# A linear-attention block with two MLPs: the diagonal term as one factor per token and head, and outputs first in the first five rounds

## The chip, the cores and the metric

The kernel runs on one core of a Trainium2 chip. The metric is the time of one execution in device microseconds. It computes everything in float32 or in float32 split into a high and a low part.

## The reference

For each batch b (2), head h (8) and time step t (768) a state of 48x48 decays and is added to; then two MLP blocks follow. Cut to what matters:

```python
for t in range(S):
    cur = einsum('bhd,bhe->bhde', u * kt, vt)
    y[:, :, t] = einsum('bhd,bhde->bhe', rt, state + cur)
    state = wt[..., None] * state + einsum('bhd,bhe->bhde', kt, vt)
h = gelu(x @ w_in); u, v = h[..., :512], h[..., 512:]
v_s = einsum('ts,bsd->btd', w_sg, layernorm(v) * g_ln) + b_sg[None, :, None]
x = x + (u * v_s) @ w_out
u = x + (relu(x.T @ w_tok1) @ w_tok2).T      # per batch
out = u + relu(u @ w_ch1) @ w_ch2
```

The term with `cur` is the diagonal: at step t it adds `sum_d(r*u*k)` of this token and head, one number, times the 48 values of v.

## The kernel before

The sequence is cut into 12 chunks of 128 tokens (NCH), six per batch (NC). In each chunk the recurrence becomes matmuls: suffix products of w scale k (`kp`, by `backward` and `scale_k`), prefix products scale r (`rp`, by `forward` and `scale_r`). TensorE then computes the scores of a chunk (`scores`), turns kp into rows (`turn_kp`), computes what the chunk adds to the state (`state_products`) and the outputs (`outputs`), which are masked scores times v plus, for all but a batch's first chunk, the old state (`sbd`) times rp. The diagonal goes by TensorE too: `diagonal(n)` there multiplies `rk` = r*k by a block matrix `ubd` of u, 12 matmuls of 32 columns each, so that each head's number stands in all of its 48 rows; VectorE multiplies this by a turned copy of v into `t1`, and its `y_tile` adds `t1` to the outputs.

The program is written out by hand, one row of instructions per engine, with semaphores between. One round is one chunk. In rounds 0 to 4 (below YR = 5) nothing of the MLPs runs: ten range checks of w (`check_range`, on ScalarE) must first be counted (`sum_range` on TensorE, `count_range` on VectorE), upon which GpSimd branches and sets `flag`. From round 5 on, products of the first MLP stand between the chunk's matmuls (table SLOT; `u`, `v` and `sg` are its products with w_in and w_sg), and TAIL has all others. ScalarE evacuates v and u with gelu and makes the high halves of split operands (`xt_high`, `split_high`), GpSimd the low ones (`xt_low`, `split_low`), in the order of their rows in the program. In rounds 0 to 4 ScalarE's iteration n is `take_k(n)` (copies the turned kp into `kn`), `take_state(n-1)` (two copies of the state into `sbd`), the checks of `checks[n]`, `xt_high(n-2)`. `keep_busy` runs matmuls of no use while the first loads are under way.

An engine's instruction waits for its semaphores and holds up everything behind it on that engine:

```python
checks = {0: (2,), 1: (3, 4), 2: (5, 6), 3: (7, 8), 4: (9,)}
def take_k(n):
    act.wait_ge(kn_turned, states(n))
    if n:
        act.wait_ge(ds_done, states(n - 1))
```

## Time and profile before

| | us |
|---|---|
| median of 3 runs (384.88 to 390.32) | 386.17 |
| profiled execution | 387.06 |
| its span, first to last instruction | 385.6 |
| busy: TensorE, GpSimd, VectorE, ScalarE | 364.2, 176.3, 163.2, 105.9 |
| mean granted clock of TensorE | 0.987 of 2.4 GHz |

The profile is of one execution. The busy time is a mean over stages with different limits: in the first 42 us VectorE is nearly always busy, from about 49 us on TensorE is. A timeline row gives an instruction or a run of like ones with its start, its length and, in brackets, the idle time ahead of it on this engine with what ended it. A matmul in float32 leaves two records, a transpose one; their ends are modelled, so the pace is read from start to start. The clock is granted at one of two levels, 2.4 or 1.2 GHz, shown as 1.0 and 0.5.

### The profile page before, as it was taken

What the parts mean: (1) busy time and instruction counts of PE and PEld (TensorE: products, weight loads), DVE (VectorE), ACT (ScalarE), POOL (GpSimd) and SP (SyncE); (2) the same over time, 40 slices, a digit from 0 to 9 for tenths busy, and PEclk for the clock granted to TensorE, in tenths of its full rate; (3) what the DMA queues carried; (4) which work ended last, traced back from release to release, by engine and by line L of the source; (5) the groups of instructions that cost most, each with busy time, mean ns of one, the idle gap of its engine ahead of it and who ended that gap; (6) DMA issues with size and microseconds to landing.
All of it is one profiled execution on the core that took longest, in us unless ns stands there. A gap on an engine that the chain in (4) does not pass through costs nothing.

```text
span 385.6 us, 7208 instructions
## 1 busy us (share of the span) xinstructions
PE 364.2 (94%) x2926; PEld 323.6 (84%) x2926; DVE 163.2 (42%) x293; ACT 105.9 (27%) x197; POOL 176.3 (46%) x181
## 2 busy tenths in 40 slices
PE   6875889999599999999999999999999999999996
PEld 5754778899599989999999999888888888888885
DVE  7997469885044414123432677331013310133110
ACT  4566425565140018340000334320012300033000
POOL 6776499999539998635999930000000000000000
PEclk9999899999799999999999999999999999999999
DMA  8999639821202020030214300000100001000001
GB/s 226 288 310 276 194 111 243 242 92 43 83 2 82 2 81 2 3 82 2 82 43 125 122 2 2 0 0 3 53 27 2 0 0 56 27 0 2 0 30 53
DMA packets 13954, 28.82 MB, mean 75 GB/s; under 512 B 1888, under 2 KB 6496, under 8 KB 13920
## 3 DMA queue, kind: packets, MB, share of 16 engines
q1 hardware_dynamic: 13920, 28.34, 25.3%
q8 instruction: 24, 0.39, 0.4%
q14 instruction: 10, 0.08, 0.1%
HBM read 25.98 MB, written 2.36 MB: 73 GB/s over the span
## 4 chain that ended last, share of the span: by engine, by line
PE 84%; issue 1%; ACT 1%; DVE 1%; DVEq 0%; ACTq 0%
PE bank L1109 77%; PE bank L1188 3%; PE bank L1205 1%; PE bank L1129 1%; PE bank L1239 1%; PE bank L1139 1%; PE bank L1151 1%; ACT uT L779 0%; ACT sg_hi L835 0%; ACT win_hi L835 0%; DVE bank L962 0%; ACT xT_hi L816 0%; DVE xr L962 0%; DVE xr L1043 0%; DVE st L954 0%
## 5 line engine op out<-in xcount | busy, mean ns | idle before, releaser
L790 ACT ACTIVATE ha_hi<-bank 128x512 fp32r<-128x512 f32 x36 | 21.5, 598 | 100.5 <-PE bank L1109 100.5
L1035 DVE SCALAR_TENSOR_TENSOR ha_lo<-bank,ha_hi 128x512 fp32r<-128x512 f32 x36 | 24.9, 692 | 49.7 <-ACT ha_hi L790 49.7
L1109 PE MATMUL bank<-u2T_hi,c_hi 128*128 128x512 f32 x108 | 42.1, 389 | 0.0
L1109 PE MATMUL bank<-u2T_lo,c_hi 128*128 128x512 f32 x108 | 42.0, 389 | 0.0
L1109 PE MATMUL bank<-ha_hi,c_lo 128*128 128x512 f32 x108 | 42.0, 389 | 0.0
L1109 PE MATMUL bank<-ha_lo,c_hi 128*128 128x512 f32 x108 | 42.0, 389 | 0.0
L1109 PE MATMUL bank<-ha_hi,c_hi 128*128 128x512 f32 x108 | 42.0, 389 | 0.0
L1109 PE MATMUL bank<-u2T_hi,c_lo 128*128 128x512 f32 x108 | 42.0, 389 | 0.0
L1109 PE MATMUL bank<-sg_hi,z_lo 128*128 128x384 f32 x96 | 33.5, 349 | 4.1 <-issue 4.1
L1109 PE MATMUL bank<-sg_hi,z_hi 128*128 128x384 f32 x96 | 33.2, 346 | 0.0
L1109 PE MATMUL bank<-sg_lo,z_hi 128*128 128x384 f32 x96 | 33.2, 346 | 0.0
L1044 DVE TENSOR_TENSOR xr<-bank,xr 128x512 f32<-128x512 f32 (+1 forms) x9 | 5.9, 661 | 57.9 <-PE bank L1109 57.9
L1109 PEld LDWEIGHTS bank<-ha_hi,c_lo 128*128 128x128 f32 x108 | 20.3, 188 | 4.2
L1109 PEld LDWEIGHTS bank<-ha_lo,c_hi 128*128 128x128 f32 x108 | 20.3, 188 | 4.2
L1109 PEld LDWEIGHTS bank<-u2T_lo,c_hi 128*128 128x128 f32 x108 | 20.3, 188 | 4.2
L1109 PEld LDWEIGHTS bank<-u2T_hi,c_lo 128*128 128x128 f32 x108 | 20.3, 188 | 4.2
L1109 PEld LDWEIGHTS bank<-u2T_hi,c_hi 128*128 128x128 f32 x108 | 20.3, 188 | 4.2
L1109 PEld LDWEIGHTS bank<-ha_hi,c_hi 128*128 128x128 f32 x108 | 20.3, 188 | 4.1
L574 POOL TENSOR_TENSOR c_lo<-raw,c_hi 128x768 fp32r<-128x768 f32 x12 | 23.1, 1928 | 1.0
L1109 PEld LDWEIGHTS bank<-sg_hi,z_lo 128*128 128x128 f32 x96 | 18.8, 196 | 4.6 <-issue 4.6
L1020 DVE SCALAR_TENSOR_TENSOR tmp<-bank,gln,bsg 128x384 f32<-128x384 f32 x16 | 9.9, 617 | 24.5 <-PE bank L1109 21.5
L538 POOL TENSOR_SCALAR gt_hi<-tmp 128x384 fp32r<-128x384 f32 x16 | 9.5, 592 | 21.7 <-DVE tmp L1024 21.7
(136 smaller groups left out, 838.0 us busy)
## 6 DMA issues: line engine op xcount, KB each, us to landing
krT<-in_kr_turned SPq DMA_DIRECT2D x12, 448.0 KB, 8.7
vn<-in_v_both SPq DMA_DIRECT2D x12, 416.0 KB, 9.6
raw<-in_moe_w_ch SPq DMA_DIRECT2D x12, 384.0 KB, 3.1
raw<-in_moe_w_sg SPq DMA_DIRECT2D x6, 384.0 KB, 4.6
out<-xr SPq DMA_DIRECT2D x8, 256.0 KB, 2.0
raw<-in_moe_w_in SPq DMA_DIRECT2D x4, 384.0 KB, 12.4
raw<-in_moe_w_tok SPq DMA_DIRECT2D x4, 384.0 KB, 3.5
wz<-in_w_turned SPq DMA_DIRECT2D x6, 225.8 KB, 7.9
```

Source lines behind the costliest of these rows:

```text
L538: return nc.gpsimd.tensor_scalar(dst, src, 1.0, 1.0, ALU.mult, ALU.mult)
L574: gp.tensor_tensor(lo, raw_view(piece, hi), hi.bitcast(F32), ALU.subtract).then_inc(w_split, 1)
L790: sc.activation(ha[0][:, i, :], bank[:, :], ACT.Relu).then_inc(act_out, 1)
L1020: ve.scalar_tensor_tensor(tmp[:, i % 2, :], bank[:, 0:HALF], gln[:, dt:dt + 1], bsg[:, at_], ALU.mult, ALU.add).then_inc(dve_out, 1)
L1035: ve.scalar_tensor_tensor(ha[1][:, i, :], bank[:, :], 0.0, ha[0][:, i, :].bitcast(F32), ALU.max, ALU.subtract).then_inc(dve_out, 1)
L1044: ve.tensor_tensor(dst[:, done:WIDE], bank[:, done:WIDE], dst[:, done:WIDE], ALU.add).then_inc(dve_out, 1)
L1109: ins = te.matmul(dst, left[l], right[r], start=first and l == 1, stop=last and (l, r) == (0, 0))
L1129: ins = te.matmul(bs[i][:, tile(p)], kp[q, n % 2, p, :], rp[q, n % RR, p, :], start=True, stop=True)
L1139: ins = te.transpose(b2[:, QP * p:QP * p + QP], kp[0:QP, n % 2, p, :], ident[0:QP, 0:QP])
L1151: ins = te.matmul(b1[q, D * p:D * p + D], kn[:, p, q], vn[:, n % VR, QP * p + HP * i:QP * p + HP * i + D], start=True, stop=True)
L1188: ins = te.matmul(yb[32 * g:32 * g + 32, tile(a)], left, right, start=first, stop=last)
L1205: ins = te.matmul(dg_bank(n)[32 * g:32 * g + 32, tile(a)], ubd[0:QP, p, 32 * j:32 * j + 32], rk[0:QP, n % 2, p, :], start=True, stop=True)
```

## The change

- The diagonal. TensorE's `diagonal(n)` is now 4 matmuls with `rk` as the stationary side and 2 columns of `ubd` as the moving one. They give one number per token and head (8 columns, `dg_cols`). VectorE multiplies v by it, spread over 48 columns each, into `vd`. TensorE adds `vd` to the outputs by three full 128x128 matmuls against the identity, at the head of `outputs(n)`, into the same accumulation. `y_tile` and `t1` are gone; in rounds 0 to 4 ScalarE's new `take_y` copies the outputs to `xr`, later `x_tile` reads the bank itself. The second, turned copy of v is no longer loaded: a transfer of v has 256 KB instead of 416 KB.
- Scores and masked scores have two buffers each in these rounds, so `mask(n)` waits for the outputs of n-2.
- The order in rounds 0 to 4. On TensorE: outputs(n), state_products(n), diagonal(n+1), scores(n+1), turn_kp(n+1); before: scores(n), turn_kp(n), diagonal(n), state_products(n), outputs(n). On ScalarE: take_y(n-1), take_state(n-1), take_k(n+1), checks[n].
- The tables. v(0,0) moves from round 5 to 6 and every later job of SLOT by one place; sg(0,0) moves to the head of TAIL. GpSimd makes kp and rp of chunk 6 right after `flag`, ahead of the low halves of w_in pieces 2 and 3, and rp of chunk 0 comes from GpSimd instead of VectorE. The warm-up is 14 narrow and 22 full matmuls instead of 54 narrow ones.

```diff
@@ -39,13 +39,15 @@
...
-DUMMIES = 54
+NARROW, FULL = 14, 22
...
-VW = NP * QP
+VP = 2 * HP
+VW = NP * VP
...
+DCOL = NP * D
...
@@ -66,15 +68,15 @@
...
 SLOT = {
-    5: [("u", 0, 0), ("u", 0, 2), ("v", 0, 0)],
-    6: [("v", 0, 1), ("v", 0, 2)],
-    7: [("v", 0, 3), ("v", 0, 4)],
-    8: [("v", 0, 5), ("u", 0, 4)],
-    9: [("u", 0, 6), ("u", 0, 1)],
-    10: [("u", 0, 3), ("u", 0, 5)],
-    11: [("u", 0, 7), ("sg", 0, 0)],
+    5: [("u", 0, 0), ("u", 0, 2)],
+    6: [("v", 0, 0), ("v", 0, 1)],
+    7: [("v", 0, 2), ("v", 0, 3)],
+    8: [("v", 0, 4), ("v", 0, 5)],
+    9: [("u", 0, 4), ("u", 0, 6)],
+    10: [("u", 0, 1), ("u", 0, 3)],
+    11: [("u", 0, 5), ("u", 0, 7)],
 }
-TAIL = ([("sg", 0, i) for i in range(1, 8)] + [("v", 1, i) for i in range(6)] + [("out", 0, i) for i in range(6)]
+TAIL = ([("sg", 0, i) for i in range(8)] + [("v", 1, i) for i in range(6)] + [("out", 0, i) for i in range(6)]
...
@@ -338,20 +340,20 @@
...
-        heads, b1, b2, bs, by = ps[0][0:QP, 0:RUN // 2], ps[1], ps[2], ps[3:5], ps[5]
-        bc = b2[:, 0:CHECKS]
-
-        def y_bank(n):
-            return ps[6] if n < YR and n % 2 else by
+        heads, b1, b2, by = ps[0][0:QP, 0:RUN // 2], ps[1], ps[2], ps[5]
+        bc = ps[7][:, 0:CHECKS]
+
+        def dg_cols(n):
+            return b1[:, DCOL:DCOL + H] if n else ps[3][:, 0:H]
+
+        def score_banks(n):
+            return ps[6:8] if n < YR and n % 2 == 0 else ps[3:5]
...
@@ -668,9 +670,8 @@
...
                 gp.tensor_copy(flag[:, :], nhalf[:, :]).then_inc(flagged, 1)
+                scale(YR + 1)
                 split_low("w_in", 2)
-                split_low("w_in", 3)
-                scale(YR + 1)
                 for n in range(YR, NCH):
                     chunk(n)
...
@@ -698,7 +699,7 @@
...
-            scale_k(0)
+            scale(0)
...
@@ -802,6 +803,11 @@
...
+            def take_y(n):
+
+                act.wait_ge(av_done, n + 1)
+                sc.copy(x_cols(n), tiles(by)).then_inc(y_done, 1)
...
@@ -834,31 +840,34 @@
...
-            high = {4: [("w_in", 0), ("w_in", 2)], 5: [("w_in", 3)], 6: [("w_in", 1)], 7: [("w_sg", 0), ("w_sg", 1)],
-                    8: [("w_sg", 2)], 9: [("w_sg", 3)], 10: [("w_sg", 4)], 11: [("w_sg", 5)]}
+            high = {4: [("w_in", 0), ("w_in", 2)], 5: [("w_in", 3)], 6: [("w_in", 1)], 7: [("w_sg", 0)], 8: [("w_sg", 1)],
+                    9: [("w_sg", 2)], 10: [("w_sg", 3), ("w_sg", 4)], 11: [("w_sg", 5)]}
...
-            for q, e in ((slice(0, D), slice(0, D)), (slice(HP, QP), slice(D, 2 * D))):
-                sc.copy(ubd[q, :, e], ucol[q, :].rearrange("q (p a) -> q p a", a=1).to_broadcast([D, NP, D])
-                        ).then_inc(u_made, 1)
+            for q, e in ((slice(0, D), 0), (slice(HP, QP), 1)):
+                sc.copy(ubd[q, :, e:e + 1], ucol[q, :].rearrange("q (p a) -> q p a", a=1)).then_inc(u_made, 1)
...
             checks = {0: (2,), 1: (3, 4), 2: (5, 6), 3: (7, 8), 4: (9,)}
+            take_k(0)
             for n in range(YR):
-                take_k(n)
                 if n:
+                    take_y(n - 1)
                     take_state(n - 1)
+                if (n + 1) % NC < NC - 1:
+                    take_k(n + 1)
                 for i in checks[n]:
                     check_range(i)
                 if n > 1:
                     xt_high(n - 2)
                 for piece in high.get(n, ()):
                     split_high(*piece)
+            take_y(YR - 1)
             take_state(YR - 1)
             for n in range(YR, NCH):
-                if n % NC < NC - 1:
+                if n > YR and n % NC < NC - 1:
                     take_k(n)
...
@@ -919,26 +928,22 @@
...
-            def scale_first_r():
-
-                wait_ring(dve, krT_in, 0)
-                dve.wait_ge(pre_done, 1)
-                ve.tensor_tensor(rp[0:QP, 0], krT[0][0:QP, 1], runs(pre, 0), ALU.mult).then_inc(rp_done, 1)
...
             def diagonal(n):
 
                 wait_ring(dve, v_in, n)
                 dve.wait_ge(dg_done, n + 1)
-                if n:
-                    dve.wait_ge(y_done, n)
-                ve.tensor_tensor(t1[:, :], dg_bank(n)[:, 0:C], vn[:, n % VR, VW:VW + C], ALU.mult).then_inc(t1_done, 1)
+                if n > 1:
+                    dve.wait_ge(av_done, n - 1)
+                ve.tensor_tensor(vd[:, n % 2, :].rearrange("s (p i d) -> s p i d", p=NP, i=2),
+                                 dg_cols(n).rearrange("s (p i a) -> s p i a", p=NP, a=1).to_broadcast([PART, NP, 2, D]),
+                                 vn[:, n % VR, :].rearrange("s (p i x) -> s p i x", p=NP, i=2)[:, :, :, 0:D], ALU.mult).then_inc(vd_done, 1)
...
             def mask(n, i):
 
                 dve.wait_ge(qk_done, n + 1)
-                if n:
-                    dve.wait_ge(av_done, n)
-                ve.tensor_tensor(am[:, :, :].rearrange("s (p i) t -> s i p t", i=2)[:, i, :, :], pairs(bs[i]),
+                if n > 1:
+                    dve.wait_ge(av_done, n - 1)
+                ve.tensor_tensor(am[:, n % 2].rearrange("s (p i) t -> s i p t", i=2)[:, i, :, :], pairs(score_banks(n)[i]),
...
@@ -954,18 +959,11 @@
...
-            def y_tile(n):
-
-                dve.wait_ge(av_done, n + 1)
-                dve.wait_ge(t1_done, n + 1)
-                src = tiles(y_bank(n))
-                ve.tensor_tensor(x_cols(n) if n < YR else src, src, tiles(t1), ALU.add).then_inc(y_done, 1)
...
             def x_tile(n):
 
                 if n == YR:
                     dve.wait_ge(flagged, 1)
-                dve.wait_ge(y_done, n + 1)
+                dve.wait_ge(av_done, n + 1)
...
@@ -1057,17 +1055,16 @@
...
             backward(0)
             forward(0)
-            scale_first_r()
             backward(1)
             forward(1)
             for n in range(YR):
                 mask(n, 0)
                 mask(n, 1)
+                if n == 0:
+                    diagonal(0)
                 backward(n + 2)
                 forward(n + 2)
-                if n:
-                    y_tile(n - 1)
-                diagonal(n)
+                diagonal(n + 1)
                 if n == YR - 1:
                     count_range()
                 state(n)
@@ -1075,19 +1072,16 @@
...
                 for b, i in v_jobs(n):
                     stats(b, i)
-                diagonal(n)
-                y_tile(n)
                 x_tile(n)
+                if n + 1 < NCH:
+                    diagonal(n + 1)
                 if n % NC < NC - 1:
                     state(n)
-            take_job("sg", 0, 0)
...
@@ -1121,8 +1115,11 @@
...
-                if n:
-                    pe.wait_ge(masked, 2 * n)
+                if n > 1:
+                    pe.wait_ge(masked, 2 * (n - 1) if n <= YR else 2 * n)
+                if n == 1:
+                    pe.wait_ge(vd_done, 1)
+                bs = score_banks(n)
...
@@ -1145,10 +1140,11 @@
...
                 if n:
                     pe.wait_ge(st_done, states(n - 1))
+                    pe.wait_ge(vd_done, n + 1)
...
@@ -1158,11 +1154,12 @@
...
                 if n > YR:
                     pe.wait_ge(x_out, n - YR)
-                elif n == YR:
+                elif n:
                     pe.wait_ge(y_done, n)
-                elif n >= 2:
-                    pe.wait_ge(y_done, n - 1)
-                inner, yb = n % NC > 0, y_bank(n)
+                inner = n % NC > 0
+                pe.wait_ge(vd_done, n + 1)
+                for a in range(KC):
+                    te.matmul(by[:, tile(a)], vd[:, n % 2, tile(a)], ident[:, :], start=a == 0, stop=False)
                 if inner:
                     pe.wait_ge(sbd_done, 2 * states(n - 1))
                 pe.wait_ge(masked, 2 * (n + 1))
@@ -1172,20 +1169,20 @@
...
-                        here = old + [(vn[:, n % VR, c:c + 32], am[:, h, :]) for c, h in new]
-                        todo += [(a, left, right, e == 0, e == len(here) - 1) for e, (left, right) in enumerate(here)]
+                        here = old + [(vn[:, n % VR, c:c + 32], am[:, n % 2, h, :]) for c, h in new]
+                        todo += [(a, left, right, a == KC - 1 and e == len(here) - 1) for e, (left, right) in enumerate(here)]
...
-                            a, left, right, first, last = part
-                            ins = te.matmul(yb[32 * g:32 * g + 32, tile(a)], left, right, start=first, stop=last)
+                            a, left, right, last = part
+                            ins = te.matmul(by[32 * g:32 * g + 32, tile(a)], left, right, start=False, stop=last)
...
@@ -1195,22 +1192,17 @@
...
-                    pe.wait_ge(t1_done, n)
-                if n >= YR:
-                    pe.wait_ge(kn_copied, states(n))
-                    pe.wait_ge(ok_counted, 1)
-                for a in range(KC):
-                    for g in range(4):
-                        p, j = divmod(4 * a + g, 3)
-                        ins = te.matmul(dg_bank(n)[32 * g:32 * g + 32, tile(a)], ubd[0:QP, p, 32 * j:32 * j + 32],
-                                        rk[0:QP, n % 2, p, :], start=True, stop=True)
-                        yield
+                    pe.wait_ge(vd_done, n)
+                    if n > 1:
+                        pe.wait_ge(st_done, states(n - 2))
+                for p in range(NP):
+                    ins = te.matmul(dg_cols(n)[:, 2 * p:2 * p + 2], rk[0:QP, n % 2, p, :], ubd[0:QP, p, :], start=True, stop=True)
                 ins.then_inc(dg_done, 1)
...
             def sum_range():
 
                 pe.wait_ge(checked, CHECKS)
-                pe.wait_ge(kn_copied, states(YR - 1))
+                pe.wait_ge(masked, 2 * YR)
                 te.matmul(bc, ones[:, :], acc[:, :], start=True, stop=True).then_inc(ok_summed, 1)
...
@@ -1291,10 +1281,12 @@
...
-            def keep_busy(m):
-
-                for i in range(m):
+            def keep_busy(narrow, full):
+
+                for i in range(narrow):
                     te.matmul(ps[6][32 * (i % 4):32 * (i % 4) + 32, 0:PART], ident[:, 0:32], ident[:, :], start=True, stop=True)
+                for i in range(full):
+                    te.matmul(ps[6][:, 0:PART], ident[:, :], ident[:, :], start=True, stop=True)
...
@@ -1302,25 +1294,31 @@
...
-            keep_busy(DUMMIES)
+            keep_busy(NARROW, FULL)
+            scores(0)
+            turn_kp(0)
+            diagonal(0)
             for n in range(YR):
-                scores(n)
-                turn_kp(n)
-                rest_of(diagonal(n))
-                rest_of(state_products(n))
                 if n == YR - 1:
                     sum_range()
                 rest_of(outputs(n))
+                rest_of(state_products(n))
+                diagonal(n + 1)
+                scores(n + 1)
+                if (n + 1) % NC < NC - 1:
+                    turn_kp(n + 1)
             for n in range(YR, NCH):
-                scores(n)
-                if n % NC < NC - 1:
-                    turn_kp(n)
+                if n > YR:
+                    scores(n)
+                    if n % NC < NC - 1:
+                        turn_kp(n)
                 for job in round_jobs(n):
                     product(*job)
-                rest_of(diagonal(n))
                 rest_of(outputs(n))
                 if n % NC < NC - 1:
                     rest_of(state_products(n))
+                if n + 1 < NCH:
+                    diagonal(n + 1)
             for job in TAIL:
...
@@ -1354,10 +1352,9 @@
...
-        t = a.reshape(B, NP, 2, NC, PART, D).transpose(0, 3, 4, 1, 2, 5).reshape(NCH, PART, NP, 2, D)
-        t = _np.concatenate([t[..., 0, :], _np.zeros_like(t[..., 0, :HP - D]), t[..., 1, :]], axis=3)
-        c = a.reshape(B, H, NC, PART, D).transpose(0, 2, 1, 4, 3).reshape(NCH, KC, PART, PART).transpose(0, 2, 1, 3)
-        return _np.concatenate([t.reshape(NCH, PART, VW), c.reshape(NCH, PART, C)], axis=2)
+        t = a.reshape(B, H, NC, PART, D).transpose(0, 2, 3, 1, 4).reshape(NCH, PART, H, D)
+        t = _np.concatenate([t, _np.zeros_like(t[..., :HP - D])], axis=3)
+        return _np.ascontiguousarray(t.reshape(NCH, PART, VW))
...
```

TensorE's row in the program from the last of outputs(1) to the first of outputs(2), before (L1188 is outputs, L1129 scores, L1139 turn_kp, L1205 the old diagonal, L1151 state products):

```order
L1188 MATMUL bank<-rp,sbd 32x128
L1188 MATMUL bank<-am,vn 32x128 x4
L1129 MATMUL bank<-rp,kp 128x128 x8
L1139 MATMUL bank<-ident,kp 128x112 x4
L1205 MATMUL bank<-rk,ubd 32x128 x12
L1151 MATMUL bank<-vn,kn 64x48
```

And of the change, from the last state products of chunk 1 on (L1147 is state products, L1199 the new diagonal, L1126 scores, L1134 turn_kp, L1162 the injects of vd, L1185 outputs):

```order
L1147 MATMUL bank<-vn,kn 64x48
L1147 MATMUL bank<-vn,kn 48x48
L1199 MATMUL bank<-ubd,rk 128x2 x4
L1126 MATMUL bank<-rp,kp 128x128 x8
L1134 MATMUL bank<-ident,kp 128x112 x4
L1162 MATMUL bank<-ident,vd 128x128 x3
L1185 MATMUL bank<-rp,sbd 32x128 x4
L1185 MATMUL bank<-am,vn 32x128 x4
```

Scores and turn_kp of chunk 2 now stand behind outputs and state products of chunk 1, and the injects of chunk 2 stand behind turn_kp(2).

ScalarE's row before, from take_k(1) on (L732 is take_k, L740 and L741 take_state, L758 and L760 checks, L816 xt_high):

```order
L732 COPY kn<-bank 128x448
L740 COPY sbd<-st 48x4x48
L741 COPY sbd<-st 48x4x48
L758 ACTIVATE junk,ok<-wz,ok 112x1024
L760 ACTIVATE junk,ok<-wz,ok 112x1024
L732 COPY kn<-bank 128x448
L740 COPY sbd<-st 48x4x48
L741 COPY sbd<-st 48x4x48
L758 ACTIVATE junk,ok<-wz,ok 112x1024
L760 ACTIVATE junk,ok<-check_w,ok 128x1152
L816 CAST xT_hi<-xr 128x3x128
```

And of the change, from take_k(0) and take_k(1) on (L733 is take_k, L809 take_y, L741 and L742 take_state, L759 and L761 checks):

```order
L733 COPY kn<-bank 128x448 x2
L761 ACTIVATE junk,ok<-wz,ok 112x1024
L809 COPY xr<-bank 128x3x128
L741 COPY sbd<-st 48x4x48
L742 COPY sbd<-st 48x4x48
L733 COPY kn<-bank 128x448
L759 ACTIVATE junk,ok<-wz,ok 112x1024
L761 ACTIVATE junk,ok<-wz,ok 112x1024
L809 COPY xr<-bank 128x3x128
L741 COPY sbd<-st 48x4x48
L742 COPY sbd<-st 48x4x48
L733 COPY kn<-bank 128x448
```

The first two `kn` copies are take_k(0) and take_k(1); take_y(0) and take_state(0) now stand behind take_k(1) and a check, where take_state(0) stood behind take_k(1) alone; from take_y(1) on there is a pair of checks in between.

## Rows read from the trace of the kernel before

**Rows 1.** The page: TensorE's busy time, share of the span, instructions.
```profile
PE 364.2 (94%) x2926; PEld 323.6 (84%) x2926; DVE 163.2 (42%) x293; ACT 105.9 (27%) x197; POOL 176.3 (46%) x181
```

**Rows 2.** Timeline of VectorE: start us, length us, engine, line, operation, tiles, shapes.
```profile
21.23 1.28 DVE L941 TENSOR_TENSOR am<-bank,cmask 128x512 f32<-128x512 f32 x2
...
25.08 0.53 DVE L962 TENSOR_TENSOR xr<-bank,t 128x384 f32<-128x384 f32 x1
...
26.88 1.28 DVE L941 TENSOR_TENSOR am<-bank,cmask 128x512 f32<-128x512 f32 x2
```

**Rows 3.** Timeline of TensorE; in brackets the idle time before, and its releaser.
```profile
8.59 1.16 PE L1129 MATMUL bank<-rp,kp 48*128 48x128 f32 x16 [2.02 <-DVE rp L926]
...
30.48 0.41 PE L1205 MATMUL bank<-rk,ubd 112*32 112x128 f32 x4 [2.47 <-issue]
...
39.05 0.77 PE L1151 MATMUL bank<-vn,kn 128*64 128x48 f32 x11 [3.17 <-issue]
...
49.34 0.47 PE L1109 MATMUL bank<-win_hi,xT_lo 128*128 128x512 f32 x1 [1.85 <-issue]
```

**Rows 4.** The chain of waits in order of time: start us, us, what.
```profile
61.42 0.59 PE bank L1151 x14
62.01 1.09 PE bank L1129 x16
63.11 0.53 PE bank L1139 x4
63.64 4.14 PE bank L1109 x18
67.78 0.79 PE bank L1205 x24
68.57 1.54 PE bank L1188 x56
...
80.56 3.17 PE bank L1109 x18
...
97.76 3.58 issue
101.34 6.10 PE bank L1109 x18
```

**Rows 5.** Timeline of ScalarE in round 3.
```profile
27.27 0.53 ACT L732 COPY kn<-bank 128x448 f32<-128x448 f32 x1 [2.15 <-PE bank L1139]
27.70 0.35 ACT L740 COPY sbd<-st 48x192 f32<-48x192 f32 x1
...
28.45 1.26 ACT L758 ACTIVATE junk<-check_w,ok 128x1152 bf16<-128x1152 f32 x1
...
31.08 0.50 ACT L816 CAST xT_hi<-xr 128x384 fp32r<-128x384 f32 x1
```

**Rows 6.** Timeline of GpSimd.
```profile
25.20 1.00 POOL L611 TENSOR_TENSOR xT_lo<-xr,xT_hi 128x384 fp32r<-128x384 f32 x1 [2.47 <-ACT xT_hi L816]
...
28.43 1.28 POOL L585 TENSOR_TENSOR rk<-krT 112x512 f32<-112x512 f32 x1
...
41.63 0.18 POOL L670 COPY flag<-nhalf 128x1 f32<-128x1 f32 x1 [1.04 <-DVE oki L979]
...
47.44 1.80 POOL L574 TENSOR_TENSOR win_lo<-raw,win_hi 128x768 fp32r<-128x768 f32 x1 [3.85 <-ACT win_hi L835]
...
99.44 1.81 POOL L574 TENSOR_TENSOR sg_lo<-raw,sg_hi 128x768 fp32r<-128x768 f32 x1
```

**Rows 7.** Weight loads by form up to 110 us: count, busy us, mean ns.
```profile
L1129 PEld LDWEIGHTS bank<-rp,kp 48*128 48x128 f32 x192 | 11.7, 187 | 3.7 <-issue 3.5
...
L1205 PEld LDWEIGHTS bank<-rk,ubd 112*32 112x32 f32 x288 | 7.4, 109 | 8.2 <-issue 7.4 <-POOL rk L585 0.4
```

**Rows 8.** Timeline of TensorE at the first transposes of x1t.
```profile
168.92 2.13 PE L1239 MATMUL bank<-ident,xr 128*128 128x128 f32 x18
```

**Rows 9.** A stretch: us, busy PE, PEld, DVE, ACT, POOL, granted clock, DMA.
```profile
39.60:43.03 3.43, 3.43 (x66) 2.90 (x61) 1.17 (x6) 1.21 (x3) 2.39 (x3) 0.58 0.69 210
```

More of the change, by code:

```diff
@@ L182, in build @@
     suf = put("suf", [PART, 2, RUN + 4])
-    vn = put("vn", [PART, VR, VW + C])
+    vn = put("vn", [PART, VR, VW])
     pre = put("pre", [PART, RUN + 4])
@@ L187, in build @@
     kn = put("kn", [PART, NP, QP])
-    am = put("am", [PART, H, PART])
+    am = put("am", [PART, 2, H, PART])
     sbd = put("sbd", [PART, 2, NP, 2 * D])
     st = put("st", [PART, NP, D])
-    t1 = put("t1", [PART, C])
+    vd = put("vd", [PART, 2, C])
     ucol = put("ucol", [PART, NP])
-    ubd = put("ubd", [PART, NP, 2 * D])
+    ubd = put("ubd", [PART, NP, 2])
     cmask = put("cmask", [PART, PART])
@@ L252, in build @@
         table_in = sem("table_in")
[L253 removed]
+        rp_done, rk_done, vd_done, flagged = sem("rp_done"), sem("rk_done"), sem("vd_done"), sem("flagged")
         xt_hi, xt_split, u2_hi, u2_split = sem("xt_hi"), sem("xt_split"), sem("u2_hi"), sem("u2_split")
@@ L391, in load_v @@
                     sp.wait_ge(ds_done, states(n - VR))
-                    sp.wait_ge(t1_done, n - VR + 1)
+                    sp.wait_ge(vd_done, n - VR + 1)
                 sp.dma_start(vn[:, n % VR, :], v_both[n]).then_inc(v_in[n % VR], 16)
@@ L435, in _ @@
             load_raw(2)
-            later = {5: [3], 6: [4, 5], 7: [6], 8: [7], 9: [8], 10: [9, 10], 11: [11, 12, 13, 14]}
+            later = {5: [3], 6: [4, 5], 7: [6], 8: [7], 9: [8], 10: [9], 11: [10, 11, 12, 13, 14]}
             for n in range(4, NCH):
@@ L641, in split_gated @@
                                  ).then_inc(g_split, 1)
-            low = {6: [("w_in", 1)], 7: [("w_sg", 0), ("w_sg", 1)], 8: [("w_sg", 2)], 9: [("w_sg", 3)],
-                   10: [("w_sg", 4)], 11: [("w_sg", 5)]}
+            low = {5: [("w_in", 3)], 6: [("w_in", 1)], 7: [("w_sg", 0)], 8: [("w_sg", 1)], 9: [("w_sg", 2)],
+                   10: [("w_sg", 3), ("w_sg", 4)], 11: [("w_sg", 5)]}
             def scale(n):
@@ L1077, in _ @@
                 mask(n, 1)
-                if n == YR:
-                    y_tile(n - 1)
                 if n + 2 < NCH:
@@ L1174, in parts @@
                         p, j = divmod(4 * a + g, 3)
-                        v0 = QP * p + 32 * j
+                        v0 = VP * p + 32 * j
                         old = [(sbd[0:QP, n % 2, p, 32 * j:32 * j + 32], rp[0:QP, n % RR, p, :])] if inner else []
@@ L1224, in free_bank @@
                 elif JOB[job][0] < EARLY:
-                    pe.wait_ge(ok_counted, 1)
-                    pe.wait_ge(y_done, YR - 1)
-                    pe.wait_ge(t1_done, YR)
+                    pe.wait_ge(masked, 2 * YR)
                 else:
```

7 lines of the change are left out of this document (1 added, 6 removed).

## The prediction

> **What bounds the kernel now.** I read the page first: TensorE (PE) is busy 94% of a span of 385.6 us, so what is left to move is what keeps PE waiting or makes it slow [rows 1]. The profiled execution took 387.06 us, 1.5 more than its span; the median of the runs is 386.17.
>
> The first 42 us are not PE's. VectorE (DVE) runs without a hole from mask(2) at 21.23 to mask(3) at 26.88, 5.65 us a round; y_tile at 25.08 is 0.53 of it [rows 2]. PE waits inside its rounds: 2.47 us before 30.48 and 3.17 us before 39.05, both put down to issue [rows 3]. After the second wait the clock was granted at 0.58 between 39.60 and 43.03, that is, mostly at 1.2 GHz instead of 2.4 [rows 9]. The fifth round ends with GpSimd (POOL) setting `flag` at 41.63, behind DVE's count of the range [rows 6]. Call this moment F: before it no product of the MLP may start.
>
> From F on the chain of waits is nearly all PE, and one round reads: state products 0.59, scores 1.09, turning 0.53, two v products 4.14, the old diagonal 0.79, outputs 1.54; two u products are 3.17 [rows 4]. There is one hole, 3.58 us at 97.76, while POOL ends the splits of `w_sg`, and behind it sg(0,0) takes 6.10 us for 18 matmuls of the shape that the u products do in 3.17: the clock is at its low level again [rows 4]. sg(0,1) starts at 101.34 + 6.10 + 0.79 + 1.54 = 109.77, 68.1 us after F. From there PE has no hole worth naming, and the change leaves that part alone.
>
> So the time after is 387.06 plus the shift of F, plus the change of the 68.1 us.
>
> **The change part by part.** *Round 0 to 4, the new order.* The order of ScalarE (ACT) is what matters most. Outputs(n) now wait for take_y(n-1) and take_state(n-1) on ACT. These stand behind take_k(n) and the range checks of iteration n-1. Take_k(n) waits for turn_kp(n), which stands in PE's row behind scores(n), diagonal(n), state_products(n-1) and outputs(n-1). This closes a loop through both engines with nothing running in parallel: turn_kp(n), take_k(n), checks, take_y, take_state, outputs(n), state products(n), diagonal(n+1), scores(n+1), turn_kp(n+1). Before, the checks stood behind take_state and hence behind what outputs waited for, in the shadow of DVE's 5.65 us.
>
> Prices of ACT's half: take_k to the next copy 0.43 (27.27 to 27.70), the two copies of take_state 0.75, a pair of checks 2.63 (28.45 to 31.08), so 1.3 for one, and xt_high 0.5 [rows 5]. Take_y is new there, a copy of 128x384 like xt_high; of each 0.45 counts, up to the next start. With 0.1 for the hand-over to PE, round 1 (one check) is 0.43+1.3+0.45+0.85 = 3.0 us, round 2 (two checks) 4.3, round 3 (and xt_high) 4.8.
>
> Prices of PE's half: outputs 1.54, state products 0.59, scores 1.09, turning with the hand-over 0.64 [rows 4], and the new diagonal. This is 4 matmuls (8 records) whose moving side is 2 columns and whose stationary side is 128, so the weight loads set it. No row shows this alone. Below: the state products' 16 records in 0.59 us, 37 ns each with 48 to 64 columns to load [rows 4], 0.3 us. Above: 8 loads of 187 ns one behind the other, 1.5 us. Loads of 32 and of 128 columns last 109 and 187 ns [rows 7], 0.8 ns for each further column, so 128 columns cost 0.10 us and with a little overhead 0.11: 0.9 us, which I take. PE's half is then 1.54+0.59+0.9+1.09+0.64 = 4.76.
>
> Start: scale_r(0) goes to POOL behind scale_k(0), and the warm-up is 14 narrow and 22 full matmuls instead of 54 narrow. Scores(0) began at 8.59 [rows 3]; kp(0) and rp(0) are now ready at about 8.2, the wider warm-up may hold PE until 10.7 if the clock is low for most of it, and I take 9.2. From there scores 1.09, turning 0.53, diagonal 0.9, VectorE's vd 0.9 with both hand-overs, inject 0.75, outputs(0) 0.88, state products 0.59, diagonal 0.9, scores 1.09, turning 0.64: T1 = 17.5, where Tn is the end of turn_kp(n).
>
> T2 = 17.5+3.0+4.8 = 25.3. T3 = 25.3+4.3+4.8 = 34.4. In round 3 POOL comes in: rk(4) stands behind xt_low(0) and scale(4). Before, from the xT_lo row at 25.20 to the start of rk at 28.43 are 3.2 us, and rk itself is 1.28 [rows 6]; xt_high(0) starts at T3+3.05 and takes 0.55, so rk(4) ends (0.55+0.1+3.2+1.28) at T3+8.15, and diagonal(4) starts there instead of at T3+6.9. T4 = 34.4+8.2+0.9+1.09+0.64 = 45.2. Round 4: PE's sum_range stands ahead of outputs(4) and waits for check 9, which is behind a pair of checks, xt_high(1), take_y and take_state: 45.2+0.43+2.6+0.45+0.45+0.75+1.4 = 51.3. Then sum 0.5, inject 0.75, outputs 1.54, state products 0.59, diagonal 0.9: 55.6; VectorE's vd 0.65 and count 0.6; POOL 0.7 later: F = 57.5. It was 41.63: **+15.9 us**. A round of 8 to 11 us stands where 5.65 stood, although DVE is rid of y_tile's 0.53 and PE's issue waits (2.47, 3.17) have room to vanish in it. What hid the checks was DVE's 5.65; that cover is gone.
>
> *The clock.* PE now idles some 3.5 us in round 2, 4 in round 3 and 6 in round 4. The wait of 3.17 us brought the low level in the trace, that of 2.47 did not. A stretch of 3.4 us at 1.2 GHz costs 1.7 us of PE's work; in round 3 it mostly hides behind POOL. I add **+3.4** for rounds 2 and 4; the bounds are 0 and 7, the latter if the low level lasts as it did at sg(0,0), 2.9 us lost each time.
>
> *After F.* PE per round: the old diagonal goes (-0.79), the new one comes (+0.9), and three full 128x128 matmuls against the identity in fp32 (6 records). The x1t transposes are full 128x128 too: 18 in 2.13 us, of which 0.27 is the last one's own length, so 0.109 us from one to the next [rows 8]; 6 of these are 0.65, with a change of the array's shape 0.75. So +0.86 in each round. Here the notes speak against the change: the Trainium skill, TensorEngine Tiling (Array Packing), Key Properties, says that changing the tiling mode drains the engine, and the injects add one change per round. The rows show no idle time at such changes, only scores' 1.09 where 8 steps of 0.11 would be 0.9; by the rule each round would pay up to 0.2 more than my 0.1, another 1 us in all.
>
> Counting from F with POOL's new order (scale(6) 2.3, low(w_in,2) 1.8, rk 1.25, two xt_low 1.9, low(w_in,3) 1.8): v(0,0) starts at F+9.4, against 7.7 before, at 49.34 [rows 3]. Rounds 6 to 11 on PE: 4.14+0.75+0.88+0.59+0.9+1.09+0.53 = 8.9 for round 6; 9.5 for 7 and for 8; 8.6 for 9; 8.0 for 10; 3.17+0.75+1.54 = 5.5 for 11. sg(0,0) may start at F+59.4. POOL ended its last `w_sg` split at 101.25, 59.6 us after F, and 3.85 of these it waited for ACT, ahead of 47.44 [rows 6]. In its new order scale(6) fills that wait, so about 56 are left. It is done 3 us before PE asks, the hole of 3.58 us closes, PE stays at the high level and sg(0,0) takes 3.17. sg(0,1) starts at F+62.6 instead of F+68.1: **-5.5 us**.
>
> The v transfers shrink from 416 KB to 256 KB; they only were late where DVE and PE ran at the old pace, so I give nothing for it. Sum: 387.06+15.9+3.4-5.5 = 400.9, and by the median 400.
>
> **The rivals.** (1) The loop through ACT binds and the clock falls: 400. (2) It binds, the clock stays high in these rounds: 396.6. For it speaks that 2.47 us of idling did nothing; against it that 3.17 us did. (3) It binds, but small prices are too high: a diagonal at 0.55 instead of 0.9 takes 0.35 off ten times on the path, and with the high clock 393 comes out, about the edge of 2%. (4) Faster: the checks do not delay outputs, since ACT would reach take_y and take_state before PE has ended scores(n). Then VectorE sets the rounds at 5.1 us, F comes 2.7 earlier for five rounds and some 2 more for the issue waits, and with -5.5 the time is 377. It decides if ACT's half is under about 1 us; the rows make it 3 to 4.8, in program order, so I give it little. (5) The two sides cancel, within 2% in all: F would have to shift by no more than 13, which needs each round shorter than my sum by 1 us.
>
> **How the numbers follow.** (1) 0.57, (2) 0.18, (3) and (5) together 0.20, of which 0.03 lies just outside 2%, (4) 0.05. About 2% is what a measurement of this kernel can tell. Slower by over 2% means above 393.9: 0.78; within: 0.17; faster: 0.05. Range: low, 400.9 with no cost of the clock (-3.4), the diagonal cheap (-3.5) and a start 1 us sooner is 393, and two more for round errors 391; high, the clock at 7 and a diagonal at 1.2 is 407.
>
> **What would show it.** ACT's row in rounds 1 to 4 should read kn, checks, (xT_hi), xr, sbd, sbd with no gap but one ahead of kn of some 4 us; PE should wait for ACT's sbd or xr ahead of outputs; `flag` should come at 55 to 62 us instead of 41.63. After F: v(0,0) 9.4 later, no hole ahead of sg(0,0), sg(0,1) some 62.6 after F, the new diagonal at 0.9 and the injects at 0.75. The prediction is wrong if F stands under 50, or if PE's rounds after F are as short as before.

## The result and the profile after

The changed kernel takes 409.25 us (median of 4 runs, 408.65 to 412.32); the kernel before took 387.03 beside it. The ratio is 1.060, its 95% interval 1.056 to 1.065 (it is taken from fast runs alone and so is a little above the quotient of the two medians): slower, as forecast, but above the 400.0 and above the end of the range, 407. The profiled execution is 408.65 us with a span of 407.1.

The page of the changed kernel, TensorE (PE) and its clock in 40 slices of 10.2 us:

```profile
PE   8787638999999999999999999999999999999996
...
PEclk9967667999999999999999999999999999999999
```

Slices 3 to 7, from 20 to 71 us, hold the loss: the clock's digits are 6 and 7 there, and PE's busy share falls to 6 and 3 tenths in slices 5 and 6. (The digits are tenths, of full speed or of the slice.) What follows is as full as before. `flag` on GpSimd (POOL), which answers to 41.63 in [rows 6], and what it waited for:

```profile
67.22 0.18 POOL L672 COPY flag<-nhalf 128x1 f32<-128x1 f32 x1 [3.64 <-DVE oki L977]
```

F, the moment of `flag`, moved by 25.6 us and lies outside the 55 to 62 that the prediction named as its sign; from F to the start of sg(0,1), 68.1 us before, it is 64.2 (67.22 to 131.4), and what is behind differs by 0.1. So 25.6 - 3.9 - 0.1 = 21.6 is the difference of the profiled executions, 408.65 - 387.06.

ScalarE (ACT) in round 2, from its timeline, which answers to [rows 5]:

```profile
28.75 0.53 ACT L733 COPY kn<-bank 128x448 f32<-128x448 f32 x1 [7.94 <-PE bank L1134]
29.31 1.15 ACT L759 ACTIVATE junk<-wz,ok 112x1024 bf16<-112x1024 f32 x1
...
31.73 0.46 ACT L809 COPY xr<-bank 128x384 f32<-128x384 f32 x1
32.09 0.35 ACT L741 COPY sbd<-st 48x192 f32<-48x192 f32 x1
32.47 0.35 ACT L742 COPY sbd<-st 48x192 f32<-48x192 f32 x1
```

And the rows of PE's timeline that had an idle time ahead of them, from round 1 to the sum of the range (L1162 is the inject at the head of outputs, L1206 the sum of the range):

```profile
20.30 1.62 PE L1162 MATMUL bank<-ident,vd 128*128 128x128 f32 x6 [2.18 <-issue]
...
32.29 1.62 PE L1162 MATMUL bank<-ident,vd 128*128 128x128 f32 x6 [3.57 <-issue]
...
44.06 1.62 PE L1162 MATMUL bank<-ident,vd 128*128 128x128 f32 x6 [4.09 <-issue]
...
58.69 0.60 PE L1206 MATMUL bank<-ok,ones 128*128 128x10 f32 x2 [6.14 <-ACT junk L759]
```

This is the loop that was forecast: PE stands still while ACT does kn, checks and xr, and ACT's only gap is ahead of kn. That gap is 7.94 us, where some 4 were forecast; in e2 below, at full clock, it is 5.30. The inject at 32.29 starts 0.1 us after xr ends (31.73 + 0.46), so "issue" hides a wait for xr. It does not wait for the two sbd copies, the second of which starts after it. What was not forecast is the 1.62 of the injects: they run at half the clock. Windows of the changed kernel, drawn near the edges of these stretches (columns: busy time of each engine, then the clock, the share of DMA and GB/s):

```profile
19.80:26.60 6.80, 6.30 (x83) 5.44 (x84) 1.71 (x3) 0.99 (x4) 3.59 (x3) 0.54 1.04 294
30.05:36.90 6.85, 4.61 (x69) 4.05 (x71) 2.15 (x4) 2.71 (x7) 0.00 (x0) 0.54 0.48 139
43.70:50.50 6.80, 6.43 (x84) 5.58 (x84) 1.41 (x2) 0.87 (x3) 4.47 (x4) 0.54 0.17 51
53.90:64.20 10.30, 5.51 (x79) 4.79 (x80) 2.13 (x4) 6.81 (x14) 7.24 (x6) 0.53 0.09 23
67.60:71.00 3.40, 3.34 (x12) 3.37 (x13) 2.91 (x6) 2.21 (x5) 3.21 (x3) 0.58 0.25 69
```

Five stretches at 1.2 GHz, 34 us in all, where the kernel before had one of 3.4 us ahead of F [rows 9] and one of 6.8 us behind it, at sg(0,0) (granted 0.54 from 101.06 to 107.90). The chain of waits of the changed kernel for round 3, the end of round 4, and the rounds behind F:

```profile
44.06 1.62 PE bank L1162 x6
45.68 3.15 PE bank L1185 x56
48.83 1.02 PE bank L1147 x14
...
67.66 4.69 PE bank L1103 x18
72.35 0.67 PE bank L1162 x6
73.02 1.68 PE bank L1185 x56
74.69 0.98 PE bank L1199 x8
...
128.24 6.79 PE bank L1103 x38
```

Inject 1.62 instead of 0.67, outputs 3.15 instead of 1.68, state products 1.02 instead of 0.59: 2.85 us lost in round 3 on the path. At 128.24 sg(0,0) follows without a hole, where [rows 4] had 3.58 us of waiting and a slow product; its row in the chain holds sg(0,0) and what follows it.

### The profile page after: what moved, and what is told of

Read it like the earlier page. It is cut to its first block, busy times and chain, and to the rows that moved or that the text cites. A ratio compares the mean times of both kernels' runs of the same rounds, so it can differ in the third digit from the quotient of the medians.

```text
span 407.1 us, 6871 instructions
## 1 busy us (share of the span) xinstructions
PE 384.3 (94%) x2770; PEld 345.0 (85%) x2770; DVE 157.2 (39%) x280; ACT 107.7 (26%) x202; POOL 177.5 (44%) x182
## 4 chain that ended last, share of the span: by engine, by line
PE 94%; issue 3%; ACT 1%; DVE 0%; POOL 0%; POOLq 0%; DVEq 0%; ACTq 0%
PE bank L1103 73%; PE bank L1185 6%; PE bank L1126 3%; PE bank L1162 3%; PE bank L1199 3%; PE bank L1147 2%; PE bank L1289 1%; PE bank L1134 1%; PE bank L1229 1%; ACT junk L759 1%; PE bank L1287 0%; DVE vd L937 0%; PE bank L1206 0%; POOLq L716 0%; DVE xr L1041 0%
## 5 line engine op out<-in xcount | busy, mean ns | idle before, releaser
L1103 PE MATMUL bank<-sg_hi,z_lo 128*128 128x384 f32 x96 | 32.3, 336 | 0.0
L1103 PE MATMUL bank<-sg_hi,z_hi 128*128 128x384 f32 x96 | 32.1, 334 | 0.0
L1103 PE MATMUL bank<-sg_lo,z_hi 128*128 128x384 f32 x96 | 32.1, 334 | 0.0
L613 POOL TENSOR_TENSOR xT_lo<-xr,xT_hi 128x384 fp32r<-128x384 f32 x12 | 13.4, 1117 | 27.7 <-ACT xT_hi L822 27.7
L1162 PE MATMUL bank<-ident,vd 128*128 128x128 f32 x72 | 13.2, 332 | 10.6 <-issue 9.8
L1185 PE MATMUL bank<-am,vn 128*32 128x128 f32 x384 | 22.0, 318 | 0.0
```

Source lines behind the costliest of these rows:

```text
L613: gp.tensor_tensor(lo, x_cols(g), hi.bitcast(F32), ALU.subtract).then_inc(xt_split, 1)
L1103: ins = te.matmul(dst, left[l], right[r], start=first and l == 1, stop=last and (l, r) == (0, 0))
L1162: te.matmul(by[:, tile(a)], vd[:, n % 2, tile(a)], ident[:, :], start=a == 0, stop=False)
L1185: ins = te.matmul(by[32 * g:32 * g + 32, tile(a)], left, right, start=False, stop=last)
```

## Experiments

**Is it the loop through ScalarE?** e1_take_k puts take_k(n) behind take_state(n-1), as the kernel before had it.

```diff
-                if (n + 1) % NC < NC - 1:
-                    take_k(n + 1)
+                if n:
+                    take_k(n)
```

> The changed kernel with one line of ScalarE's order in rounds 0 to 4 altered: behind take_state(n-1) stands take_k(n) instead of take_k(n+1), so the checks no longer stand between a turn_kp and the outputs that follow it. If the loop through ScalarE is what costs (theory): a round is turning, 0.7 for the inject, outputs 1.68, state products 0.6, diagonal 0.98, scores 1.09, turning 0.53, about 5.6 us instead of 10.6 to 12.6, no idle of over 2 us before outputs, the clock stays high until round 4, flag comes at about 45 us instead of 67.2, and the time is about 387. If the outputs-first order of TensorE or the new diagonal's price is what costs (rival): 400 or more.

390.46 us (ratio 1.016, 1.008 to 1.024), `flag` at 48.73 instead of 67.22. VectorE's masks (L946) now come every 5.98 us, in its timeline:

```profile
26.18 1.28 DVE L946 TENSOR_TENSOR am<-bank,cmask 128x512 f32<-128x512 f32 x2
...
31.02 0.56 DVE L937 TENSOR_TENSOR vd<-bank,vn 128x384 f32<-128x384 f32 x1 [0.91 <-PE bank L1199]
...
32.16 1.28 DVE L946 TENSOR_TENSOR am<-bank,cmask 128x512 f32<-128x512 f32 x2
```

One moved line takes off 18.8 of the 22.2 us by the medians, or 4.4 of the 6.0% by the ratios, each to the kernel before that ran beside it. The rest came in above the 387 I expected: vd waits 0.91 us a round for the new diagonal, scores(0) starts at 10.74 behind the wide warm-up, and the sum waits 2.43 us for check 9. The clock is low for short stretches too, granted at 0.51 from 14.60 to 18.00, behind a wait of 0.81 us, and at 0.50 from 42 to 45, behind the wait of the sum.

e3_small_checks shortens the same half of the loop in another way: checks 2 to 9 read 8 columns, so most of the range check is left out.

```diff
+                if i > 1:
+                    src, dst = (src[:, 0:1, 0:8], dst[:, 0:1, 0:8]) if i < NC else (src[:, 0:8], dst[:, 0:8])
```

> The changed kernel with checks 2 to 9 reading 8 columns of w instead of 1024 or 1152; their number, order and semaphores stay. It leaves out most of the range check. A check falls from 1.28 to some 0.45 us. If the checks in the loop are the cover that was lost (theory), the eight of them give back 6.6 us, and more (up to 8) where the idle before outputs gets short enough for the clock to stay high: 394 to 403. If the loop binds by something else on ScalarE or GpSimd (rival): 408 to 410.

400.24 us (1.044, 1.031 to 1.057), `flag` at 57.64, 9.6 us earlier, and the idle times ahead of the injects are 1.33, 1.88 and 2.29. That checks delay outputs is shown. The clock still fell in four of five rounds: behind the wait of 1.33 us it was granted at 0.51 from 19.50 to 22.80.

**Is the rest the clock?** e2_fill puts matmuls of no use where PE waits for ACT, 9, 15, 17 and 26 of them behind turn_kp(1) to turn_kp(4); nothing on ACT's side changes.

```diff
                 if (n + 1) % NC < NC - 1:
                     turn_kp(n + 1)
+                    for _ in range(FILL[n]):
+                        te.matmul(score_banks(n)[0][:, 0:PART], ident[:, :], ident[:, :], start=True, stop=True)
```

> The changed kernel with matmuls of no use (9, 15, 17 and none, full 128x128) behind turn_kp(1) to turn_kp(4), 26 behind the last, in the wait for ScalarE; the order is left alone. If the low clock is what made the rounds longer than their sum at the high clock (theory): the injects take 0.67 instead of 1.6, outputs 1.7 instead of 3.1, the rounds 7.8, 9.1 and 10.8 instead of 10.6, 11.3 and 12.6, and the time is 400 to 402. If ScalarE's half is longer than I priced it and the clock matters little (rival): 408 to 410.

403.58 us (1.050, 1.042 to 1.058); `flag` at 59.51, 7.7 us earlier with more work on PE. The profiled execution, 401.06 us, is 7.6 below that of the changed kernel; the median is above the 400 to 402 that I expected. PE's idle rows in it:

```profile
20.04 0.91 PE L1163 MATMUL bank<-ident,vd 128*128 128x128 f32 x6 [0.15 <-issue]
...
39.28 0.91 PE L1163 MATMUL bank<-ident,vd 128*128 128x128 f32 x6 [0.28 <-issue]
43.44 1.05 PE L1200 MATMUL bank<-ubd,rk 112*128 112x2 f32 x8 [0.99 <-POOL rk L588]
```

The injects are at full speed, and the wait for GpSimd's rk(4), which the prediction had put into round 3, shows once PE is fast.

e8_fill_first fills only the first wait, the one of 2.18 us: FILL is (9, 0, 0, 0).

> The changed kernel with filler matmuls only in round 1 (9 full matmuls behind turn_kp(1)), so that TensorE does not idle the 2.18 us ahead of the injects of outputs(1). Theory (each idle stretch brings its own 6.8 us at 1.2 GHz): the low stretch from 19.8 to 26.6 us goes and the later three stay, flag comes some 2.5 us earlier than 67.2, the time is 405.5 to 407.5. Rival (the low level comes from the whole of rounds 0 to 4 being lightly used, and one filled wait is made up by an earlier or longer low stretch): as many low stretches as before, flag within 1 us of 67.2, 408.5 to 410.

406.93 us (1.055, 1.047 to 1.063), `flag` at 63.35, 3.9 us earlier; 0.3 of these were there already at scores(0) (9.38 instead of 9.69). The first stretch of its windows, and PE's row at the second wait:

```profile
19.80:26.60 6.80, 5.82 (x107) 5.09 (x106) 3.73 (x8) 1.45 (x5) 3.60 (x3) 1.00 1.04 330
```

```profile
29.34 1.62 PE L1163 MATMUL bank<-ident,vd 128*128 128x128 f32 x6 [3.57 <-issue]
```

The first fence is the window, the second PE's row. The clock is 1.00 where it was 0.54; the second wait, untouched, still brings an inject at 1.62, and the third one does too (40.58). So each wait brings its own stretch. Not all of the 3.9 us reached the end, 2.4 of them did in the profiled executions: behind F the low stretch moved from the first u pair (3.38 us instead of 4.69) to the v pair (5.95 instead of 4.13), and ahead of that stands an issue wait of 0.95.

**Would another order of PE close the loop elsewhere?** e4_scores_first puts diagonal(n+1), scores(n+1), turn_kp(n+1) ahead of outputs(n).

```diff
-                rest_of(outputs(n))
-                rest_of(state_products(n))
                 diagonal(n + 1)
                 scores(n + 1)
                 if (n + 1) % NC < NC - 1:
                     turn_kp(n + 1)
+                rest_of(outputs(n))
+                rest_of(state_products(n))
```

> The changed kernel with TensorE's order in rounds 0 to 4 turned back in part: diagonal(n+1), scores(n+1), turn_kp(n+1), then outputs(n), state_products(n), and state products wait for vd(n+1) since they share its bank; ScalarE's order is left as the change has it. Theory: take_k(n+1) then waits for the state products of n, the loop is take_k 0.5, a pair of checks 2.6, xt_high 0.45, take_y and take_state 1.2, outputs 1.7, state products 0.6, some 7.2 us a round instead of 11.3, and the idle before outputs is short enough for the high clock: about 394 to 398. Rival, that TensorE's order is of no account beside ScalarE's: 405 or more.

A miss: 412.35 us (1.071, 1.062 to 1.079), `flag` at 71.12. The rival's number came true, but TensorE's order is of account: it made things worse. PE's timeline in it:

```profile
47.80 1.87 PE L1199 MATMUL bank<-ubd,rk 112*128 112x2 f32 x8 [8.29 <-POOL rk L587]
65.42 1.87 PE L1199 MATMUL bank<-ubd,rk 112*128 112x2 f32 x8 [8.42 <-POOL rk L587]
```

rk stands behind xt_low on GpSimd, xt_low waits for xt_high, which stands behind the checks on ACT, and these behind take_k. The loop closes through three engines; I had followed only two.

**What stands behind F?** e5_old_pool is e1 with GpSimd's order of before behind `flag` (low halves of w_in pieces 2 and 3 ahead of scale(6)).

> The kernel of e1_take_k with GpSimd's order behind flag as it was before the change: the low halves of w_in pieces 2 and 3 first, then kp and rp of chunk 6, and no split in chunk 5. It isolates the new order on GpSimd. Theory of the prediction, that scale(6) ahead of the splits is needed to fill GpSimd's wait: scores(6) and all behind it start later or GpSimd ends its splits later, a hole opens ahead of sg(0,0), 391 to 398. Rival: since the high half of piece 3 is early now, the wait is gone either way, v(0,0) starts some 1.8 us earlier than the 10.1 us after flag, and the time is 388 to 389.

391.62 us (1.013, 1.010 to 1.016), not to be told from e1's. It lies in the range of the theory, but without its hole. The wait behind `flag` that the prediction built on, 3.85 us ahead of a half of w_in [rows 6], does not come back, it is 0.52; a wait of 3.85 stands later, ahead of a half of w_sg, and e1 has one of 3.58 in that place. PE has no hole ahead of sg(0,0): the first fence is GpSimd's timeline, the second the chain.

```profile
52.25 1.83 POOL L576 TENSOR_TENSOR win_lo<-raw,win_hi 128x768 fp32r<-128x768 f32 x1 [0.52 <-ACT win_hi L842]
...
83.84 1.83 POOL L576 TENSOR_TENSOR sg_lo<-raw,sg_hi 128x768 fp32r<-128x768 f32 x1 [3.85 <-ACT sg_hi L842]
...
108.28 1.84 POOL L576 TENSOR_TENSOR sg_lo<-raw,sg_hi 128x768 fp32r<-128x768 f32 x1
```

```profile
109.60 1.68 PE bank L1186 x56
111.28 0.89 PE bank L1104 x4
```

The last split ends 60.4 us after `flag`, in e1 60.0, and sg(0,0) starts 1.2 us behind it. So in this kernel GpSimd's order is not what closes the hole. e7_tables_only takes the kernel before and gives it the change's tables alone (SLOT, TAIL, the orders of the splits and raw loads, and GpSimd's order behind `flag`); diagonal, rounds 0 to 4 and warm-up stay.

```diff
-    5: [("u", 0, 0), ("u", 0, 2), ("v", 0, 0)],
-    6: [("v", 0, 1), ("v", 0, 2)],
+    5: [("u", 0, 0), ("u", 0, 2)],
+    6: [("v", 0, 0), ("v", 0, 1)],
...
-TAIL = ([("sg", 0, i) for i in range(1, 8)]
+TAIL = ([("sg", 0, i) for i in range(8)]
```

> The kernel before with the change's tables alone: SLOT and TAIL (sg(0,0) at the head of TAIL), GpSimd's order behind flag, the tables of high and low halves and of raw loads. The diagonal, the order of rounds 0 to 4 and the warm-up stay as before. Theory: flag stays at about 41.6, the hole of 3.6 us and the low clock at sg(0,0) go, and with the old diagonal (0.79 us a round instead of 0.98+0.67) sg(0,1) starts some 60 us after flag instead of 68: 378 to 382. Rival, that the hole closed only because flag came so late that loads and splits were ready: 385 or more.

382.48 us (0.988, 0.981 to 0.994): the tables are the good part of the change, though `flag`, at 43.55, came 1.9 us later than before. Its chain has, in place of 3.58 us of waiting and 6.10 of a slow sg(0,0):

```profile
98.36 1.54 PE bank L1186 x56
99.90 1.86 issue
101.75 10.32 PE bank L1107 x58
```

PE comes to sg(0,0) 56.4 us after `flag`, about as before (56.1), but with outputs(11) behind it by then, and GpSimd's last split ends 58.1 us after `flag` instead of 59.6. The products behind the wait of 1.86 us ran at full clock.

e6_diag_twice measures the new diagonal alone: it is issued twice for chunks 7 to 11.

```diff
-                for p in range(NP):
+                for p in tuple(range(NP)) * (2 if n > YR + 1 else 1):
```

> The changed kernel with the four matmuls of the new diagonal issued twice for chunks 7 to 11, where TensorE has no hole. If one diagonal is worth the 0.98 us that stands between its start and the next one's in the trace, five more cost 4.9 us: 413.5 to 415. If weight loads of 128 columns hide under other work as the trace of the kernel before would allow (0.3 us), 1.5 us: about 410.8. An inject would cost nothing more in either.

417.14 us (1.080, 1.071 to 1.089), more than either expected. Its chain of waits:

```profile
94.68 1.88 PE bank L1199 x16
...
98.18 5.71 PE bank L1103 x18
...
118.31 1.64 PE bank L1126 x16
```

And two of its windows:

```profile
98.00:100.00 2.00, 2.00 (x7) 1.56 (x6) 2.00 (x4) 1.92 (x4) 0.00 (x0) 0.55 0.00 0
118.60:122.00 3.40, 3.40 (x25) 3.17 (x22) 2.28 (x5) 1.76 (x4) 3.40 (x4) 0.51 0.23 89
```

Two diagonals are 1.88, so a further diagonal costs 0.90 and the first 0.98: five make 4.5 us of the 8.1 by which the span grew. The rest is the clock: behind two of the five double diagonals it fell for 3.4 us with PE busy all the time. The v pair took 5.71 instead of 4.13, and in the other place scores, turning and a u pair 1.6 more. With 0.4 by which `flag` was later that is the 8.1.

**A version that beats both?** b1 is e1 with check 9 in iteration 3, xt_high ahead of the checks, the count ahead of diagonal(5) on VectorE, and 12 full matmuls in the warm-up instead of 22.

```diff
-NARROW, FULL = 14, 22
+NARROW, FULL = 14, 12
...
-            checks = {0: (2,), 1: (3, 4), 2: (5, 6), 3: (7, 8), 4: (9,)}
+            checks = {0: (2,), 1: (3, 4), 2: (5, 6), 3: (7, 8, 9), 4: ()}
...
-                diagonal(n + 1)
                 if n == YR - 1:
                     count_range()
+                diagonal(n + 1)
```

> The kernel of e1_take_k with check 9 in iteration 3, xt_high ahead of the checks, VectorE's count of the range ahead of diagonal(5), and 12 full warm-up matmuls instead of 22. Theory: TensorE's 2.4 us wait ahead of the range sum and the low clock behind it go, flag no longer waits for outputs(4), state products and diagonal(5), and comes at 41 to 44 us instead of 48.7: 384 to 388. Rival: the product cannot start before scores(5) are done anyway, and the time stays within 1.5 us of e1_take_k's.

383.67 us (0.992, 0.988 to 0.996), `flag` at 41.03, as in the kernel before. Four things changed at once, and none of them is priced alone. b2 moves diagonal(n+1) ahead of outputs(n) too, and vd(n+1) behind the masks:

> The kernel of b1 with diagonal(n+1) ahead of outputs(n) on TensorE and vd(n+1) right behind the masks on VectorE, so that VectorE does not wait 0.9 us a round for it. Theory: the rounds fall from 5.98 us to 5.1 to 5.3, some 3 us less than b1: 381 to 385. Rival: rk(n+1) from GpSimd comes too late for the earlier place in rounds 2 to 4, and nothing or less is gained.

A miss again: 388.64 us (1.004, 1.002 to 1.006). In the profiled execution, the slowest of the ten (391.34), PE waits for GpSimd at once:

```profile
12.81 1.05 PE L1199 MATMUL bank<-ubd,rk 112*128 112x2 f32 x8 [2.14 <-POOL rk L587]
```

c1 puts b1's checks, xt_high and count on e7:

> The kernel before with the changed tables (382.5 us when it ran) and three more steps off the path to the flag: check 9 with those of round 3, the high half of x ahead of the checks, the count of the range ahead of the diagonal on VectorE. In that run the count waited 1.37 us for TensorE's sum, which waited for check 9. Theory: flag comes 1.5 to 2.5 us earlier than 43.55 and the time is 380 to 381.5. Rival: a late issue of TensorE or the low clock in rounds 1 to 4 sets the flag, and it stays within 1 us: 382 to 383.5.

381.96 us (0.989, 0.985 to 0.992), not to be told from e7. The theory missed; the rival's time is near, but `flag` came 1.5 us later than in e7 and not within 1. The profiled execution is the slowest of the ten (384.45), and GpSimd's timeline in it shows a third reason:

```profile
42.74 1.82 POOL L574 TENSOR_TENSOR win_lo<-raw,win_hi 128x768 fp32r<-128x768 f32 x1
45.01 0.18 POOL L670 COPY flag<-nhalf 128x1 f32<-128x1 f32 x1 [0.45 <-issue]
```

`flag` no longer waits for the count but stands behind a split on its own engine. Issue waits of 3.74 and 2.31 us on PE in rounds 2 and 3 stand ahead of that; that they made it late is argued, not shown. The fastest kernels here, c1, e7 and b1, are 1.1, 1.2 and 0.8% faster than before. That is less than 2%, though each interval lies below 1, and the runs do not rank the three. The first two keep the old diagonal.

## Why the prediction was wrong in size

**The loop: right.** With the waits filled (e2) the loop can be read without the clock: kn starts at 17.91, 25.86, 35.22 and 46.15, and 17.5, 25.3, 34.4 and 45.2 were forecast for T1 to T4. Two errors in it cancelled, by luck. The inject (0.67) was left out of PE's half of 4.76, where it belongs in every round; and the two state copies (0.75) were charged to ACT's half, though they run under the inject, since only the products behind it read the state: kn at 28.75 to the inject at 32.29 is 3.5 us, not 4.3. Round 4 from kn to the sum, 6.1, came out as forecast (52.59 to 58.69). In e2 the 26 matmuls held the sum up, to 7.25 us; with 6.1 its F would be 58.4, and 57.5 was forecast.

**The clock: the step that failed.** It was priced at +3.4 with a bound of 7, for rounds 2 and 4, because an idle time of 2.47 us in the kernel before had brought nothing and one of 3.17 had. Here 2.18 us in round 1 brought the low level (in e3 even 1.33 us did), and e8 shows that this first wait alone moved F by 3.9 us, or 3.6 without the earlier start. Four waits brought four stretches, of 6.8 us three times and 10.3 once, not 3.4 each. F came at 67.22 instead of 57.5 + 3.4 = 60.9; against 58.4 the clock cost 8.8 us ahead of F, where 3.4 stood (0.25 of the 8.8 is a later start than in e2, 9.69 instead of 9.44). The reading was made from two idle times, and the first wait of the changed kernel contradicts it. The row that should have warned me is sg(0,0) in [rows 4]: 2.9 us lost after one hole. I named it as a bound for two rounds instead of taking it for all four.

That round 3 would hide its part behind GpSimd failed too: in the changed kernel rk(4) ended at 48.17 and the slow outputs at 48.8, so PE itself was late.

**The sum.** The loop gave 0.9 us more than forecast, the clock 5.4 and the part behind F 1.6, less 0.1 behind sg(0,1): together the 7.8 us between 400.9 and the profiled execution's 408.65.

**After F: -3.9 instead of -5.5.** v(0,0) started 10.1 us behind F, not 9.4. In e8, with the first u pair at full clock (3.38 instead of 4.69), it is 9.7, so 0.4 is the slow u pair; the other 0.3 is GpSimd, which began scale(6) 0.56 us after `flag`, where its first instruction had come 0.14 after it before. From there to sg(0,1) it is 54.1 us against 53.2: outputs take 1.68 each, not 1.54, six times 0.14. The diagonal (0.9 forecast, 0.98) and the inject (0.75 forecast, 0.67) cancel. The outputs are the same 56 records as in the chain of e7, 1.54 there behind a diagonal of 32-column matmuls and 1.68 here behind a full-array inject. Inject and outputs together are 2.35 us, where my sum had 2.29. The Trainium skill, TensorEngine Tiling (Array Packing), Key Properties, says that changing the tiling mode drains the engine, and my estimate from it was up to 0.2 more than the sum, 2.49; the trace lies between, and no run separates the cause. The injects hardly add a change of shape: they are 128*128 like the products ahead of them, and outputs now have the change that the old diagonal had; the added one is the new diagonal's, between state products and scores.

The hole closed as forecast, but not for the reason given, and that is luck. GpSimd was to end its last split of `w_sg` 56 us after F, 3 ahead of PE. It ended 59.9 after F, as before (59.6), and waited for ACT at another place:

```profile
100.80 1.83 POOL L576 TENSOR_TENSOR sg_lo<-raw,sg_hi 128x768 fp32r<-128x768 f32 x1 [3.47 <-ACT sg_hi L841]
...
125.23 1.85 POOL L576 TENSOR_TENSOR sg_lo<-raw,sg_hi 128x768 fp32r<-128x768 f32 x1
```

What closed the hole is PE, which came to sg(0,0) 61.0 us after F instead of 56.1, 1.2 us behind the split. The tables put outputs(11) ahead of sg(0,0), and each round has an inject and a dearer diagonal; how much of the 4.9 us each of these gives is not shown alone.

**The rivals.** (1) was the right one; (2), the loop with a high clock, is what e2 nearly is (403.6 with its filler, where 396.6 was forecast). (3) fell with the diagonal, 0.98 and not 0.55, and (5) with F's shift of 25.6. (4) would have needed ACT's half under 1 us; it is 2.1, 3.5 and 4.1.

## What to carry to other kernels

When a reordering closes a loop between two engines, price each wait of TensorE twice: the wait itself, and the work behind it at half the clock. In the changed kernel four waits of 2.2 to 6.1 us cost some 9 us more in this way. Follow a moved step through every engine whose row it stands in, since e4 and b2 failed on a third engine, GpSimd with its rk, which stood for only 0.4 us of waiting in [rows 7]. And split a change that loses: here one line of it cost 18.8 us, while its tables alone gain 1.2%. A forecast that comes true is checked for its reason too: the hole ahead of sg(0,0) closed, and GpSimd, which was to close it, was as late as before.
